# Lower halves of h in an expert kernel: all made by VectorE in one operation from the sum, with blocks of h in another order

## What is computed

```python
def _moe2_ref(x, w_gate, w1, w2):          # x 1536x512, w1 8x512x1024, w2 8x1024x512
...
    for e in range(E):
        h = np.maximum(x @ w1[e], 0.0)
        ye = h @ w2[e]
        out += P[:, e:e + 1] * ye
    return out.astype(np.float32)
```

## Time and profile before

| | |
|---|---|
| median of 3 runs | 1301.58 us (1301.51 to 1302.0) |
| profiled execution, its own time | 1301.61 us |
| span of that execution, first to last instruction | 1299.8 us |
| mean granted TensorE clock | 0.998 of 2.4 GHz |
| PE busy | 1250.4 us, 96% |
| DVE busy | 600.8 us, 46% |
| ACT busy | 435.4 us, 33% |
| POOL busy | 710.7 us, 55% |
| L611 on POOL, 192 times | 194.9 us, mean 1016 ns |
| L1135 on ACT, 192 times | 98.0 us, mean 511 ns |

### The profile page before, as it was taken

How to read it: one execution, slowest core, us unless ns; L and a number is a source line. 1 busy time by engine, 2 the same in 40 slices (tenths; PEclk the granted TensorE clock), 3 DMA queues, 4 the chain that set the end, 5 groups by cost and what they waited for, 6 DMA issues and landing times.

```text
span 1299.8 us, 18938 instructions
## 1 busy us (share of the span) xinstructions
PE 1250.4 (96%) x6462; PEld 1097.0 (84%) x6462; DVE 600.8 (46%) x1171; ACT 435.4 (33%) x999; POOL 710.7 (55%) x768
## 2 busy tenths in 40 slices
PE   5888999999999999999999999999999999999998
PEld 3556899998888888888888888888888888888887
DVE  4886645334554444444444444444444444444444
ACT  4664544342225222222222222222222222223222
POOL 4554222675555555555555555555555555555552
PEclk9999999999999999999999999999999999999999
DMA  7661000001111111111111111111111111111102
GB/s 156 154 154 45 1 1 1 17 33 33 33 33 33 34 33 33 33 32 32 32 32 32 32 33 32 32 33 36 35 38 36 33 32 32 32 32 33 34 17 97
DMA packets 62607, 53.17 MB, mean 41 GB/s; under 512 B 9824, under 2 KB 49760, under 8 KB 62560
## 3 DMA queue, kind: packets, MB, share of 16 engines
q1 hardware_dynamic: 62560, 52.57, 14.1%
HBM read 49.40 MB, written 3.15 MB: 40 GB/s over the span
## 4 chain that ended last, share of the span: by engine, by line
PE 70%; POOL 14%; issue 10%; DVE 3%; ACT 1%; SPq 1%; POOLq 0%; DMA 0%; DVEq 0%
PE ps L729 23%; PE ps L731 22%; PE ps L730 22%; POOL ring L611 6%; POOL ring L603 5%; POOL ring L599 2%; ACT probs L978 1%; PE ps L676 1%; PE ps L658 1%; DVE probs L1209 1%; PE ps L779 1%; POOL probs L492 1%; PE ps L701 1%; PE ps L916 1%; POOL ring L589 0%
## 5 line engine op out<-in xcount | busy, mean ns | idle before, releaser
L611 POOL TENSOR_TENSOR ring<-sums,ring 128x384 fp32r<-128x384 f32 x192 | 194.9, 1016 | 413.3 <-ACT sums L1135 413.3
L1443 DVE SCALAR_TENSOR_TENSOR acc<-ps,gate_now,acc 128x512 f32<-128x512 f32 x336 | 252.2, 751 | 224.9 <-PE ps L731 224.9
L729 PE MATMUL ps<-ring 128*128 128x512 f32 x768 | 303.5, 395 | 17.3 <-POOL ring L611 14.0
L730 PE MATMUL ps<-ring 128*128 128x512 f32 x768 | 299.7, 390 | 0.0
L731 PE MATMUL ps<-ring 128*128 128x512 f32 x768 | 299.4, 390 | 0.0
L1120 ACT ACTIVATE sums<-ps 128x384 f32<-128x384 f32 x192 | 94.4, 492 | 542.0 <-PE ps L731 541.9
L1419 DVE TENSOR_TENSOR sums<-ps,sums 128x384 f32<-128x384 f32 x192 | 106.7, 556 | 259.3 <-ACT sums L1120 165.3
L729 PEld LDWEIGHTS ps<-ring 128*128 128x128 f32 x768 | 144.1, 188 | 54.8 <-issue 27.3
L731 PEld LDWEIGHTS ps<-ring 128*128 128x128 f32 x768 | 144.2, 188 | 30.9
L730 PEld LDWEIGHTS ps<-ring 128*128 128x128 f32 x768 | 144.2, 188 | 26.0
L729 PE MATMUL ps<-xw,ring 128*128 128x384 f32 x448 | 152.4, 340 | 0.5 <-ACT sums L1120 0.4
(11 more groups left out here) (140 smaller groups left out, 1722.1 us busy)
## 6 DMA issues: line engine op xcount, KB each, us to landing
w_in<-w_exp SPq DMA_DIRECT2D x64, 256.0 KB, 3.3
w_raw<-w_exp SPq DMA_DIRECT2D x64, 128.0 KB, 2.6
w_raw<-w_exp SPq DMA_DIRECT2D x32, 256.0 KB, 3.1
q_sb<-qT SPq DMA_DIRECT2D x16, 192.0 KB, 3.7
k_sb<-kT SPq DMA_DIRECT2D x16, 192.0 KB, 4.0
v_sb<-v SPq DMA_DIRECT2D x16, 192.0 KB
out<-acc SPq DMA_DIRECT2D x12, 256.0 KB, 2.0
k_sb<-kT SPq DMA_DIRECT2D x16, 128.0 KB, 3.8
```

The lines of the kernel that those rows point to most:

```text
L611: pool.tensor_tensor(h_at(1, i, b * BLK, BLK), c_sum(m), h_at(0, i, b * BLK, BLK).bitcast(F32), ALU.subtract).then_inc(h_lo_pool, 1)
L729: pe.matmul(o, ws[0], xs[0], start=first, stop=False, skip_group_check=True)
L730: pe.matmul(o, ws[0], xs[1], start=False, stop=False, skip_group_check=True)
L1443: dve.scalar_tensor_tensor(out=acc[:, T, :], in0=y_bank(u, T), scalar=gate_now[:, T:T + 1], in1=acc[:, T, :], op0=ALU.mult, op1=ALU.add).t ...
```

## The change

POOL's `rest_hidden` goes (192 L611 operations), and with it ACT's second Relu (192 L1135 operations). DVE's `rest_hidden` now makes the lower half of all four blocks. For C12 it reads PSUM as before; for C11, C22 and C21 it reads the sum from SBUF and the upper half from SBUF. One semaphore, `h_lo_out`, counts all lower halves in the order of the table HIS. C21 of half 0 is summed ahead of C11 of half 1, on DVE and in the order of ACT's Relus. On DVE the lower half of C21 of half 1 stands behind output tile 1, and that of the next unit's C11 behind output tile 10.

```diff
--- before.py
+++ after.py
@@ -251,7 +251,7 @@
         w1_sums, w1_hi, w1_split = sem("w1_sums"), sem("w1_hi"), sem("w1_split")
         w2_hi, w2_split = sem("w2_hi"), sem("w2_split")
         product_full, part_copied, c_summed = sem("product_full"), sem("part_copied"), sem("c_summed")
-        h_hi_out, h_lo_dve, h_lo_pool = sem("h_hi_out"), sem("h_lo_dve"), sem("h_lo_pool")
+        h_hi_out, h_lo_out = sem("h_hi_out"), sem("h_lo_out")
         acc_scaled = sem("acc_scaled")
         y_full, y_free = sem("y_full"), sem("y_free")
         gate_col = sem("gate_col")
@@ -321,9 +321,9 @@
         PRODUCTS = ((1, 0), (2, 0), (6, 0), (7, 0), (5, 0), (1, 1), (2, 1), (3, 0), (4, 0), (6, 1), (7, 1), (5, 1),
                     (3, 1), (4, 1))
         PARTS = ((V1, 0), (U2, 0), (W, 0), (V1, 1), (U2, 1), (W, 1))
-        SUMS = ((C11, 0), (C22, 0), (C11, 1), (C21, 0), (C22, 1), (C21, 1))
+        SUMS = ((C11, 0), (C22, 0), (C21, 0), (C11, 1), (C22, 1), (C21, 1))
         C12 = 3
-        HIS = ((C11, 0), (C22, 0), (C11, 1), (C12, 0), (C21, 0), (C22, 1), (C12, 1), (C21, 1))
+        HIS = ((C11, 0), (C22, 0), (C12, 0), (C21, 0), (C11, 1), (C22, 1), (C12, 1), (C21, 1))
 
         def nth(table, u, key):
 
@@ -604,34 +604,19 @@
                                               w2c(0, i * BANK, BANK).bitcast(F32), ALU.subtract)
                 last.then_inc(w2_split, 1)
 
-            def rest_hidden(u, m, s):
-
-                i, b = c_place(m, s)
-                pool.wait_ge(h_hi_out, nth(HIS, u, (m, s)))
-                pool.tensor_tensor(h_at(1, i, b * BLK, BLK), c_sum(m), h_at(0, i, b * BLK, BLK).bitcast(F32),
-                                   ALU.subtract).then_inc(h_lo_pool, 1)
-
             combine(0)
             sum_w1(0)
             pool.wait_ge(o_full, o_index(NB - 1, 0))
             split_w1(0, 0)
             combine(1)
-            rest_hidden(0, C11, 0)
 
             def unit(u, uu, last=False):
                 split_w2(u)
-                rest_hidden(u, C22, 0)
-                rest_hidden(u, C11, 1)
-                rest_hidden(u, C21, 0)
                 if not last:
                     sum_w1(u + 1)
-                rest_hidden(u, C22, 1)
-                rest_hidden(u, C21, 1)
-                if not last:
                     if not first(u):
                         pool.wait_ge(product_full, nth(PRODUCTS, u - 1, (4, 1)))
                     split_w1(u + 1, (uu + 1) % 2)
-                    rest_hidden(u + 1, C11, 0)
 
             for uu in range(4):
                 unit(uu, uu)
@@ -849,7 +834,7 @@
                 if first(u):
                     pe.wait_ge(o_out, o_index(2 + s, 0) if s else o_index(2, 0))
                 else:
-                    pe.wait_ge(h_lo_dve, 2 * u + (s - 1))
+                    pe.wait_ge(h_lo_out, nth(HIS, u - 1, (C12, s)))
                 product(u, uu, 1, s, a_bank(s), True)
                 if s == 1:
                     pe.wait_ge(c_summed, nth(SUMS, u, (C11, 0)))
@@ -882,13 +867,9 @@
 
                 if T == 0:
                     pe.wait_ge(w2_split, u + 1)
-                    pe.wait_ge(h_lo_pool, nth(SUMS, u, (C21, 0)))
-                if T == TPB:
-                    pe.wait_ge(h_lo_dve, 2 * u + 1)
+                    pe.wait_ge(h_lo_out, nth(HIS, u, (C21, 0)))
                 if T == 2 * TPB:
-                    pe.wait_ge(h_lo_pool, nth(SUMS, u, (C21, 1)))
-                if T == 3 * TPB:
-                    pe.wait_ge(h_lo_dve, 2 * u + 2)
+                    pe.wait_ge(h_lo_out, nth(HIS, u, (C21, 1)))
                 if isinstance(u, int) and u < 4:
                     if not (u == 0 and T < 2):
                         pe.wait_ge(y_free, NT * u + (T - 1))
@@ -1128,11 +1109,8 @@
                     act.wait_ge(c_summed, nth(SUMS, u, (m, s)))
                 if not first(u):
                     act.wait_ge(y_full, NT * u + (TPB * (b + 1) - NT))
-                if m == C12:
-                    act.activation(h_at(0, i, b * BLK, BLK), a_bank(s), ACT.Relu).then_inc(h_hi_out, 1)
-                else:
-                    act.activation(h_at(0, i, b * BLK, BLK), c_sum(m), ACT.Relu)
-                    act.activation(c_sum(m), c_sum(m), ACT.Relu).then_inc(h_hi_out, 1)
+                act.activation(h_at(0, i, b * BLK, BLK), a_bank(s) if m == C12 else c_sum(m),
+                               ACT.Relu).then_inc(h_hi_out, 1)
 
             def scale_acc(T):
                 if T == 0:
@@ -1147,10 +1125,10 @@
                 copy_part(u, W, 0)
                 copy_part(u, V1, 1)
                 relu(u, C22, 0)
-                relu(u, C11, 1)
                 relu(u, C12, 0)
                 copy_part(u, U2, 1)
                 relu(u, C21, 0)
+                relu(u, C11, 1)
                 copy_part(u, W, 1)
                 relu(u, C22, 1)
                 relu(u, C12, 1)
@@ -1413,18 +1391,18 @@
                     dve.wait_ge(product_full, nth(PRODUCTS, u, (4, s)))
                     at, part = b_bank(s), U2
                 if s == 1:
-                    dve.wait_ge(h_lo_pool, nth(SUMS, u, (m, 0)))
+                    dve.wait_ge(h_lo_out, nth(HIS, u, (m, 0)))
                 elif not first(u):
-                    dve.wait_ge(h_lo_pool, nth(SUMS, u - 1, (m, 1)))
+                    dve.wait_ge(h_lo_out, nth(HIS, u - 1, (m, 1)))
                 dve.tensor_tensor(c_sum(m), at, part_sum(part, s), ALU.add).then_inc(c_summed, 1)
 
-            def rest_hidden(u, s):
-
-                i, b = c_place(C12, s)
-                dve.wait_ge(h_hi_out, nth(HIS, u, (C12, s)))
-                dve.scalar_tensor_tensor(out=h_at(1, i, b * BLK, BLK), in0=a_bank(s), scalar=0.0,
-                                         in1=h_at(0, i, b * BLK, BLK).bitcast(F32), op0=ALU.max,
-                                         op1=ALU.subtract).then_inc(h_lo_dve, 1)
+            def rest_hidden(u, m, s):
+
+                i, b = c_place(m, s)
+                dve.wait_ge(h_hi_out, nth(HIS, u, (m, s)))
+                dve.scalar_tensor_tensor(out=h_at(1, i, b * BLK, BLK), in0=a_bank(s) if m == C12 else c_sum(m),
+                                         scalar=0.0, in1=h_at(0, i, b * BLK, BLK).bitcast(F32), op0=ALU.max,
+                                         op1=ALU.subtract).then_inc(h_lo_out, 1)
 
             def gate_column(e):
 
@@ -1446,25 +1424,34 @@
             def unit(u, uu, last=False):
                 gated = isinstance(u, int) and u < 4
                 sum_c(u, C22, 0)
+                rest_hidden(u, C22, 0)
+                rest_hidden(u, C12, 0)
+                sum_c(u, C21, 0)
+                rest_hidden(u, C21, 0)
                 sum_c(u, C11, 1)
-                rest_hidden(u, 0)
-                sum_c(u, C21, 0)
                 if gated:
                     gate_step((uu, "g"))
+                rest_hidden(u, C11, 1)
                 sum_c(u, C22, 1)
                 if uu == 0 and not gated:
                     dve.wait_ge(acc_scaled, NT)
                 add_expert(u, 0)
-                rest_hidden(u, 1)
+                rest_hidden(u, C22, 1)
+                rest_hidden(u, C12, 1)
                 sum_c(u, C21, 1)
                 for T in range(1, NT):
                     if T == NT - 2 and not last:
                         sum_c(u + 1, C11, 0)
                     add_expert(u, T)
+                    if T == 1:
+                        rest_hidden(u, C21, 1)
+                    if T == NT - 2 and not last:
+                        rest_hidden(u + 1, C11, 0)
                     if gated:
                         gate_step((uu, T))
 
             sum_c(0, C11, 0)
+            rest_hidden(0, C11, 0)
             for uu in range(4):
                 unit(uu, uu)
             with dve.Fori(1, EXPERTS - 1) as e:
```

## The result

The changed kernel takes 1309.49 us (median of 4 runs, 1309.18 to 1309.63), the kernel before 1301.79 in the same comparison (4 runs, 1301.51 to 1302.78): a ratio of 1.006, 95% interval 1.0046 to 1.0073. It is slower by 7.7 us. The profiled execution took 1309.18 us with a span of 1307.4; that of before 1301.61 and 1299.8. The granted clock was 0.997 here and 0.998 there, so it plays no part.

A forecast was written before the change was run, and what follows sets the result against it. PE was taken as the bound, with stops ahead of output tile 0 worth 25.5 us at most. Loop units +8.4, six written-out units +1.5, unit 31 -0.6: +9.3, so 1311 us; own range 1305 to 1317, 8-in-10 range 1287 to 1317.

The forecast's parts named there:

- Step 1: On POOL, sums and split of the next w1 move forward beside the new DVE operations; sums from 696.62 to 699.57.
- Step 2: DVE asks for C22 inside POOL's sum L571, ends 0.41 behind it and holds up L573 by 0.3 us.
- Step 3: POOL's split starts 0.2 us later (bounds 0.08 and 0.28); the first L589 runs from 701.88 to 703.04.
- Step 4: Ahead of output tile 0: DVE asks for C21 0.2 after L589 starts, ends at 703.45; PE wins 0.11, not 0.87.
- Step 5: Half 1: C11's sum and Relu stand behind C21, ACT copies W later, product 3 is delayed 0.1 (bounds 0 and 0.25).
- Step 6: Product 4 of half 1: its sum of C22 stands behind C11's held lower half; new stop of 0.4 (bounds 0.3 and 0.55).
- The written-out units: Units 1 to 3 and 28 to 30: same order as the loop, shorter lag to PE, +0.25 us each, +1.5 together.
- No meeting: Rival: DVE and POOL don't block each other, so the chain ends in time; -22.4 us, 1279; chance 0.12.
- DVE goes first: Rival: at C21 DVE asks just before the first L589, product 4 stops about 0.25; -14.7 us, 1287; chance 0.12.
- C11 slips through: Rival: C11's sum and Relu 0.2 faster, DVE asks before the third L589, no stop at product 4; about 1301; chance 0.07.
- Longer stops: Rival: the steps from C22 to product 4 at their upper bounds, +0.6 us a unit; 1318; chance 0.04.
- The rule on the source of the operand: New DVE operations: 62 cycles less from SBUF than PSUM, an estimated 0.06 us each, 1.9 in all; not adopted.

The follow-up runs named there:

- e1: Changed kernel with one added wait: POOL sums and splits the next w1 only after DVE made C11's lower half of half 1; 1275.46 us.
- e6: Changed kernel plus a small extra POOL operation of 64 columns between the sums and the split of w1; 1309.81 us.
- e2: Changed kernel with the lower halves of C11, C22 and C21 computed from PSUM instead of the SBUF sum, leaving out the right values; 1275.32 us.
- e11: Changed kernel plus an extra POOL operation of 192 columns between the sums and the split of w1; 1301.23 us.
- e12: Changed kernel plus an extra POOL operation of 384 columns between the sums and the split of w1; 1292.93 us.
- e4: Changed kernel where only POOL's split of w1 waits, for the lower half of C21 of half 0, and the sums stay early; 1276.71 us.

## Why the prediction was right

The forecast was 1311; it came to 1309.5, slower, in its own range. By its steps:

- **The bound.** Right: stops worth 25.5 us were the most to win. Without stops (e1) the kernel takes 1275.46, 26.0 below before.
- **Step 1, POOL's list moves forward.** Right: the whole of the sums and splits runs beside the lower halves (POOL from 699.32 to 709.74).
- **Step 2, C22 holds up L573.** Said 0.3, bounds 0 and 0.38; L573 takes 1.10 and its undisturbed twin 0.75, so 0.35.
- **Step 3, L583 0.2 later.** Right: the gap is 0.20. Filling it (e6) cost nothing.
- **Step 4, C21 refused.** The mechanism was right, the size was not. DVE asks 0.18 behind the start of L589 (said 0.2) and takes 1.38 (said 1.35). But the stop shrank by 0.21, not by 0.11. The sum had compared the ends of the two lower halves and so kept the lag of 0.24 from there to PE, which is the lag behind POOL. Behind DVE it is 706.33 - 706.19 = 0.14 here.
- **Step 5, product 3 late by 0.1.** Near the lower bound: the copy of W does come later and the weights of product 3 are loaded 0.15 late, but its matmuls only 0.02.
- **Step 6, the stop at product 4.** Right in cause and place: released by L1397 behind the refused C11, which takes 1.40 (said 1.39). The sum was ready 709.20 - 695.69 = 13.51 after L599 (said 13.49). Said 0.4, measured 0.46 in this unit, for two reasons of opposite sign: PE got here 0.16 earlier than forecast (steps 4 and 5) and so waited longer, and it started 709.25 - 709.20 = 0.05 after the sum, where 0.12 to 0.24 had been put.
- **The written-out units** were undersized, +0.25 each. The trace has this for the last ones:

```profile
1220.93 0.34 PE L716 MATMUL ps<-xw,w_b 128*128 128x384 f32 x1
1221.64 0.47 PE L714 MATMUL ps<-ring 128*128 128x512 f32 x1 [0.37 <-issue]
1221.95 0.40 PE L715 MATMUL ps<-ring 128*128 128x512 f32 x1
...
1224.60 0.44 PE L714 MATMUL ps<-xw,w_b 128*128 128x384 f32 x1 [0.29 <-DVE sums L1397]
```

  A stop of 1221.95 - 1221.33 = 0.62 ahead of tile 0 and one of 0.55 at product 4, where before had one of 0.69: +0.45 in each of the six; over the units it is 0.54 to 0.62 and 0.55, which is the 1.13 used above. The prediction made these units cheaper by their shorter lag to PE. The lag is shorter there (0.10 behind POOL before and behind DVE now, and tile 0 wins the 0.1 that was said), but the stop at product 4 is longer than in the loop, not shorter. Unit 31 came out as said: its stop of 0.70 is gone (said -0.6).
- **The sum.** Over 23 units of the loop the difference is +6.4 (32.20 against 31.93 us a unit, +0.28, where the prediction had 0.35). Up to the start of unit 4 the two traces differ by 1.0, unit 4 itself gives back 0.5 and the last four units add 0.7. Together +7.6 in the span, said +9.3. The slips of steps 4 and 5 never reach the total: product 4 waits for the sum of C22 in either case, so what PE wins ahead of tile 0 it loses there. What makes a unit cheaper than said is the lag at product 4, and unit 4; what makes the whole dearer is the written-out units. These errors have opposite signs, so the total is better than its terms, which is luck in part.
- **Unit 4** has the refusal at another point of POOL's operation, and it fits the rule that DVE waits for the rest of it. Its products take longer on PE (10.81 us from the first start to the last, 10.26 in the unit of the rows), so C21 asks 0.73 behind the start of the L589 and not 0.18, takes 0.85 and not 1.38, and the stop is 0.11. That is 0.3 of the 0.5 that this unit gives back; the rest was not traced:

```profile
414.75 5.12 POOL L589 TENSOR_TENSOR w_b<-w_raw,w_b 128x448 fp32r<-128x448 f32 x4
```

```profile
415.48 0.85 DVE L1403 SCALAR_TENSOR_TENSOR ring<-sums,ring 128x384 fp32r<-128x384 f32 x1 [1.34 <-ACT ring L1112]
```

- **The rivals.** "No meeting" (1279) is refuted by the profile (a mean of 818 ns), and e2 shows what it would have brought: the same list without refusals takes 1275. "DVE goes first" (1287) does not happen by itself; e11 brings it about in every second unit, and the point from which it decides is a lead of between 0.01 and 0.055 us. The premise for it, steps 2 and 3 longer by 0.15, missed: they were longer by 0.05. "C11 slips through" (1301) missed by 0.16, the distance from the start of the third L589 to C11's request. "Longer stops" (1318) needed +0.6 a unit; it was +0.28 in the loop and +0.45 in the written-out units.
- **The rule on the source of the operand** (the Trainium skill, "VectorE: DVE Perf Modes", the TRN2 errata; an estimated 1.9 us less by it) does not show here: undisturbed, the form with both inputs in SBUF has a median of 558 ns and that with PSUM 557.

## What to carry to other kernels

Before moving an operation to VectorE, look at which of its inputs lie in SBUF and what GpSimd runs at that moment; an operation of 0.56 us with two inputs in SBUF took up to 1.57 here beside GpSimd's of 1.15, and one with an input in PSUM took 0.56 in all 64 cases of the changed kernel and all 256 of e2. When an engine is relieved, its remaining list moves forward in time: here that brought POOL's work onto the critical operations, and one wait that held it back gave 34 us. The gain in these runs comes from where the refusal falls and not from how much of it there is: in e12 the new operations have a mean of 876 ns, more than the 818 of the changed kernel, and the kernel is 16.6 us faster. Where the work can't be moved, shorter operations on GpSimd bound the refusal, and what another engine waits for goes ahead of an operation that may be refused.

## What the runs showed of the hardware

- The refusal is decided at the start and lasts until POOL's operation ends: 1.57 us at the same recorded start, 0.56 with a lead of 0.06 (e11), 0.85 when DVE asks 0.73 us into a L589 of 1.15 (unit 4 of the changed kernel). Refused operations end 0.40 to 0.42 us after POOL's (63 cases in the changed kernel).
- Between two back-to-back operations of POOL a waiting DVE gets in. The next one of POOL is lengthened by 0.3 to 0.4 us (L589 1146 to 1472 ns and L573 1.10 against 0.75 in the changed kernel, L583 0.94 to 1.34 in e4), less than DVE's recorded 0.56. The Trainium skill ("SBUF — State Buffer", Who interferes with whom) calls the block between two such instructions a full one. For DVE the rows of e11 agree; for POOL these rows give less than DVE's recorded duration.
- From the end of the last operation to PE's first matmul ahead of tile 0 it was 0.13 to 0.14 us behind DVE and 0.24 behind POOL in the loop, but 0.10 behind either in the written-out units, and 0.05 to 0.06 behind DVE ahead of product 4 everywhere. So it is not a property of the engine alone; what sets it was not tried.
- POOL's 0.20 us between the end of L575 and L583 took up most of an added operation of 0.29 us (e6).
- Why POOL wins at equal recorded starts, and where between 0.01 and 0.055 us the turning point lies, was not tried.
